# Denominators as products of two factors, one of them in PSUM, and quotients formed in the bank of 1/Q

## The chip, the cores and the metric

The kernel runs on one core of a Trainium2 chip. Its time is device microseconds of one execution; three executions of the kernel before gave 477.53, 478.20 and 479.14 us, so the median is 478.2 us. A profiled execution of its own gave the rows below.

## The reference

Three layers run one after the other. A small attention (a pooled one added to one over a band of seven keys) gives x of 1152 tokens by 512. Then two feed-forward layers follow, each from 512 to 2048 and back to 512:

```
# layer 1
h = x @ w_in
P = a[0] + a[1] * h + a[2] * h * h + a[3] * h * h * h
Q = 1.0 + abs(b[0]) * abs(h) + abs(b[1]) * h * h
y = (P / (Q + 1e-06)) @ w_out
# layer 2
sp = where(h > 20, h, log1p(exp(minimum(h, 20))))
y = (h * tanh(sp)) @ w_out
```

With u = exp(h), tanh(log(1 + u)) is u(u + 2) / (u(u + 2) + 2), so both layers need a quotient whose denominator is D plus a constant, with D = |h|(|b0| + |b1||h|) in layer 1 and D = u(u + 2) in layer 2.

## The kernel before

**Tiles.** The feed-forward work is cut into 81 tiles, 40 in layer 1 and 41 in layer 2. A tile is 128 rows of the hidden dimension, or two such groups side by side, over a block of tokens. In layer 1 the blocks have 256, 256, 256, 192 and 192 tokens and every tile has two row groups, so a tile is 128x512 in the first three blocks and 128x384 in the last two. In layer 2 tiles are 128x512, 128x384 and then 128x512 and 128x256. All products are done as three float16 products (head times head, rest times head, head times rest).

**One tile q passes all engines.** TensorE's `hidden(q)` (L602) fills `h_bank[q % 2]`. ScalarE reads it in `first_reads` (L742 square, L745 scaled magnitude, L748 a cubic coefficient step; in layer 2 L750 the exponential). VectorE's `fraction` works in three parts: in layer 1 L915 (denominator), L922 and L929 (polynomial); in layer 2 L918, L925 (denominator) and L934. ScalarE's `estimate` (L759 logarithm, L761 exponential of its negative) puts about 1/Q in `inv_bank[q % 2]`, which is PSUM. VectorE's `quotient` makes one Newton step and the product in three parts: L943, L947, and L953 or L956. ScalarE's `head` (L769) rounds the result to float16, GpSimd's `rest` (L1061) takes what is left over, and TensorE's `output_first` (L623) or `output_second` (L643) multiplies both with the second weights.

**Order.** Each engine takes its instructions in the order written. TensorE's is output(m), hidden(m + 4), output(m + 1), and so on; hidden(q) waits until VectorE has done part 2 of fraction(q - 2) (`h_done`), output(q) waits for `rest(q)` (`g_rest`). In ScalarE's round m stand first_reads(m), head(m - 2), estimate(m). In VectorE's round m stand fraction part 0 of m, quotient part 0 of m - 1, fraction part 1 of m, quotient part 1 of m - 1, fraction part 2 of m, quotient part 2 of m - 1. Between these pieces `schedule.until(tick)` puts in the attention's pieces and the splitting of weights into head and rest (`head_unit` on ScalarE, L728; `rest_unit` on VectorE, L901, or on GpSimd, L1047 and L1049), at ticks from a table that the change leaves as it is. At the end of a block of layer 1, `leave_y` turns the output banks into the next layer's input: L777 on ScalarE, then L965 on VectorE, for which TensorE's first instruction on these banks (L617) waits.

**The attention** fills the first 55 us, and pieces of it run among the tiles until about 220 us: `put_k` (L684), `put_p` and `put_d` (L668) on ScalarE, pooling and normalising on GpSimd (L1013 to L1037).

Of the kernel before, what the change touches and what calls it, by code (L numbers as in the profile page):

```python
# [10 lines left out]
ALU = mybir.AluOpType  # L11
# [15 lines left out]
def attention_moe_moe(nc, q, k, v, w_in1, w_out1, a, b, w_in2, w_out2, out):  # L27
# [163 lines left out]
    with ExitStack() as ctx:  # L191
# [3 lines left out]
        def sem(name):  # L195
            return ctx.enter_context(nc.semaphore(name))
# [74 lines left out]
        b0_s, b1_abs = coef[:, 10:11], coef[:, 11:12]  # L271
# [35 lines left out]
        h_read = sem("h_read")  # L307
# [356 lines left out]
        def _(act):  # L664
# [68 lines left out]
            def first_reads(q):  # L733

                layer, w = tiles[q][0], width(q)
                ps = h_bank[q % 2][:, 0:w]
                act.wait_ge(h_ready, q + 1)
                if q >= 3:
                    act.wait_ge(g_done, q - 2)
                d, t = den[q % 3][:, 0:w], num[q % 4][:, 0:w]  # L740
                if layer == 0:
                    act.activation(d, ps, ACT.Square, scale=1.0 / HS)  # L742
                    if q >= 2:
                        act.wait_ge(den_done, q - 1)
                    act.activation(ab[q % 2][:, 0:w], ps, ACT.Abs, scale=b0_s).then_inc(h_read, 1)  # L745
                    if q >= 4:
                        act.wait_ge(g_rest, q - 3)
                    act.activation(t, ps, ACT.Identity, scale=a_s[3], bias=a_s[2]).then_inc(t1_done, 1)  # L748
                else:
                    act.activation(d, ps, ACT.Exp, scale=1.0 / HS).then_inc(h_read, 1)  # L750

            def estimate(q):

                layer, w = tiles[q][0], width(q)
                r = inv_bank[q % 2][:, 0:w]
                act.wait_ge(den_done, q + 1)
                if q >= 2:
                    act.wait_ge(nr_done, q - 1)
                act.activation(r, den[q % 3][:, 0:w], ACT.Ln, bias=(one_eps, two)[layer]).then_inc(ln_done, 1)  # L759
                act.wait_ge(ln_done, q + 1)  # L760
                act.activation(r, r, ACT.Exp, scale=-1.0, bias=(0.0, ln_k)[layer]).then_inc(inv_done, 1)  # L761
# [30 lines left out]
            act.activation(b1_abs, b_raw[:, 1:2], ACT.Abs).then_inc(coefs, 1)  # L792
            schedule.until(LAYERS)
            act.wait_ge(coefs, 8)
# [18 lines left out]
        def _(dve):  # L813
# [94 lines left out]
            def fraction(part, q):  # L908

                layer, w = tiles[q][0], width(q)  # L910
                h, d, t = h_bank[q % 2][:, 0:w], den[q % 3][:, 0:w], num[q % 4][:, 0:w]
                if part == 0:
                    dve.wait_ge(h_read, q + 1)
                    if layer == 0:
                        dve.scalar_tensor_tensor(out=d, in0=d, scalar=b1_abs, in1=ab[q % 2][:, 0:w],  # L915
                                                 op0=ALU.mult, op1=ALU.add).then_inc(den_done, 1)
                    else:
                        dve.tensor_scalar(d, d, EXP_20, None, ALU.min).then_inc(clamped, 1)  # L918
                elif part == 1:
                    if layer == 0:  # L920
                        dve.wait_ge(t1_done, q + 1)
                        dve.tensor_tensor(t, t, h, ALU.mult).then_inc(t2_done, 1)  # L922
                    else:
                        dve.wait_ge(clamped, q - N1 + 1)
                        dve.scalar_tensor_tensor(out=d, in0=d, scalar=2.0, in1=d, op0=ALU.add,  # L925
                                                 op1=ALU.mult).then_inc(den_done, 1)
# [10 lines left out]
            def quotient(part, q):  # L937
# [48 lines left out]
            dve.tensor_scalar(b0_s, b_raw[:, 0:1], 1.0 / HS, None, ALU.mult).then_inc(coefs, 1)  # L986
# [5 lines left out]
            dve.wait_ge(coefs, 8)  # L992
# [119 lines left out]
```

## Time and profile before

| what | value |
|---|---|
| median of three executions | 478.2 us |
| profiled execution, its own time | 478.56 us |
| its span, first to last instruction | 476.4 us |
| TensorE busy | 461.9 us, 97% |
| VectorE busy | 398.1 us, 84% |
| ScalarE busy | 306.2 us, 64% |
| GpSimd busy | 214.9 us, 45% |

The profiled execution is 2.16 us longer than its span, and 0.36 us over the median. A busy share is a mean over stages: attention up to about 55 us, layer 1 up to about 290 us, layer 2 after it.

### The profile page before, as it was taken

Reading aid. Unit: us, or ns where it says so; the run is one execution under the profiler, and the core shown is the slowest. Engines: PE = TensorE matmul, PEld = TensorE weight load, DVE = VectorE, ACT = ScalarE, POOL = GpSimd, SP = SyncE. Lnnn points to the kernel's source line nnn. Section 1 sums busy time; section 2 is a strip of 40 time slices with the busy share of each in tenths; the row PEclk is TensorE's granted clock in tenths of the full one; section 3 lists DMA queues with packets and bytes.
Section 4 is the critical chain, followed back from the end, with each engine's and each line's share of the span. In section 5 each row is a group of like instructions: output and inputs, shape, how many; then the busy total and the mean of one; then the engine's idle time right before and its main releaser. Section 6 shows DMA issues by size and latency. Waiting matters only on the chain.

```text
span 476.4 us, 11017 instructions
## 1 busy us (share of the span) xinstructions
PE 461.9 (97%) x4318; PEld 338.3 (71%) x4318; DVE 398.1 (84%) x671; ACT 306.2 (64%) x565; POOL 214.9 (45%) x224
## 2 busy tenths in 40 slices
PE   6999799999999999999999999999999999999996
PEld 5667689898889788899998976444444555557662
DVE  7787799999787887878878788998899888878894
ACT  4477578888566585678877776566545555554542
POOL 5789935579352422117422635762625122212122
PEclk8997899999999999999999999999999999999999
DMA  5989733610801100020200221132000200000101
GB/s 120 247 202 296 159 92 90 161 24 2 190 1 37 24 3 3 1 89 1 89 4 1 89 89 45 45 90 88 0 1 0 90 0 2 0 1 1 66 3 44
DMA packets 46436, 29.71 MB, mean 62 GB/s; under 512 B 31792, under 2 KB 39984, under 8 KB 46384
## 3 DMA queue, kind: packets, MB, share of 16 engines
q1 hardware_dynamic: 45168, 28.71, 22.3%
q8 instruction: 34, 0.56, 0.5%
q10 hardware_dynamic: 1216, 0.30, 0.3%
q14 instruction: 18, 0.15, 0.1%
HBM read 26.64 MB, written 2.36 MB: 61 GB/s over the span
## 4 chain that ended last, share of the span: by engine, by line
PE 77%; POOL 11%; DVE 4%; ACT 3%; issue 3%; DMA 1%; SPq 0%; ACTq 0%; POOLq 0%
PE bank L602 33%; PE bank L643 18%; PE bank L623 17%; PE bank L565 3%; POOL g_l L1061 2%; POOL w L1049 2%; PE bank L509 1%; POOL work L1047 1%; DMA late<-in_k 1%; POOL late L1013 1%; POOL late L1037 1%; POOL late L1049 1%; PE bank L552 1%; ACT late L684 1%; POOL raw L1047 1%
## 5 line engine op out<-in xcount | busy, mean ns | idle before, releaser
L1061 POOL TENSOR_TENSOR g_l<-work,g_h 128x512 f16<-128x512 f32 (+2 forms) x81 | 90.4, 1116 | 212.0 <-ACT g_h L769 179.1
L602 PE MATMUL bank<-x_h,w 128*128 128x256 f16 (+1 forms) x640 | 102.5, 264 | 2.7 <-DVE work L929 2.7
L623 PE MATMUL bank<-g_h,w 128*128 128x256 f16 (+1 forms) x640 | 101.3, 262 | 0.5 <-POOL g_l L1061 0.4
L602 PE MATMUL bank<-x_h,late 128*128 128x512 f16 (+2 forms) x384 | 96.9, 326 | 0.0
L759 ACT ACTIVATE bank<-work,coef 128x512 f32<-128x512 f32 (+2 forms) x81 | 52.3, 646 | 64.3 <-DVE work L925 63.1
L643 PE MATMUL bank<-late,g_h 128*128 128x512 f16 x288 | 92.1, 379 | 0.1
L602 PE MATMUL bank<-x_l,w 128*128 128x256 f16 (+1 forms) x320 | 84.6, 264 | 0.0
L623 PE MATMUL bank<-g_l,w 128*128 128x256 f16 (+1 forms) x320 | 83.8, 262 | 0.0
L602 PEld LDWEIGHTS bank<-x_h,w 128*128 128x128 f16 x640 | 61.4, 99 | 8.5 <-DVE work L929 2.9
L623 PEld LDWEIGHTS bank<-g_h,w 128*128 128x128 f16 x640 | 60.8, 98 | 8.1 <-issue 2.1
L602 PE MATMUL bank<-x_l,late 128*128 128x512 f16 (+2 forms) x192 | 62.6, 326 | 0.0
L602 PEld LDWEIGHTS bank<-x_h,late 128*128 128x128 f16 x384 | 37.6, 98 | 26.2
L915 DVE SCALAR_TENSOR_TENSOR work<-work,coef 128x512 f32<-128x512 f32 (+1 forms) x40 | 32.1, 803 | 27.1 <-ACT work L745 27.0
L643 PE MATMUL bank<-late,g_l 128*128 128x512 f16 x144 | 54.6, 379 | 0.0
L643 PEld LDWEIGHTS bank<-late,g_h 128*128 128x128 f16 x288 | 28.2, 98 | 33.5 <-POOL g_l L1061 1.4
L943 DVE SCALAR_TENSOR_TENSOR work<-work,bank 128x512 f32<-128x512 f32 (+2 forms) x81 | 50.1, 619 | 0.0
L947 DVE SCALAR_TENSOR_TENSOR work<-work,bank 128x512 f32<-128x512 f32 (+2 forms) x81 | 49.9, 616 | 0.0
L769 ACT ACTIVATE g_h<-work 128x512 f16<-128x512 f32 (+2 forms) x81 | 47.3, 583 | 2.5 <-DVE work L956 2.4
L925 DVE SCALAR_TENSOR_TENSOR work<-work 128x512 f32<-128x512 f32 (+2 forms) x41 | 47.1, 1150 | 0.0
L742 ACT ACTIVATE work<-bank 128x512 f32<-128x512 f32 (+1 forms) x40 | 22.2, 555 | 32.0 <-PE bank L602 26.8
L918 DVE TENSOR_SCALAR work<-work 128x512 f32<-128x512 f32 (+2 forms) x41 | 18.8, 460 | 24.6 <-ACT work L750 24.6
L602 PEld LDWEIGHTS bank<-x_l,w 128*128 128x128 f16 x320 | 31.6, 99 | 2.2
(103 smaller groups left out, 804.9 us busy)
## 6 DMA issues: line engine op xcount, KB each, us to landing
raw<-in_moe_w_in SPq DMA_DIRECT2D x10, 512.0 KB, 5.6
raw<-in_moe_w_out SPq DMA_DIRECT2D x10, 512.0 KB, 4.3
late<-in_k SPq DMA_DIRECT2D x16, 144.0 KB, 4.1
late<-in_v SPq DMA_DIRECT2D x8, 288.0 KB
late<-in_v SPq DMA_DIRECT2D x32, 72.0 KB
out<-w SPq DMA_DIRECT2D x9, 256.0 KB, 2.3
late<-in_moe_w_in SPq DMA_DIRECT2D x4, 512.0 KB, 3.6
late<-in_moe_w_out SPq DMA_DIRECT2D x4, 512.0 KB, 4.5
```

The source lines that it names most:

```text
L602: last = pe.matmul(ps, w_in(l, wp)[:, kk, at], x[:, kk, t0:t0 + n], start=(kk == 0 and wp == 0 and x is x_h), stop=(kk == KD - 1 and wp == 1))
L623: last = pe.matmul(ps, w_out(0, wp)[:, f, 128 * d:128 * (d + 1)], g[q % 4][:, i * n:(i + 1) * n], start=False, stop=(f == FT - 1 and d % 2 ...
L643: last = pe.matmul(y2_bank[row % 4][:, :], g[q % 4][:, i * n + 128 * t:i * n + 128 * (t + 1)], w_out(1, wp)[:, f, :], start=(f == 0 and wp ...
L742: act.activation(d, ps, ACT.Square, scale=1.0 / HS)
L759: act.activation(r, den[q % 3][:, 0:w], ACT.Ln, bias=(one_eps, two)[layer]).then_inc(ln_done, 1)
L769: act.activation(g_h[q % 4][:, 0:w], num[q % 4][:, 0:w], ACT.Copy).then_inc(g_head, 1)
L915: dve.scalar_tensor_tensor(out=d, in0=d, scalar=b1_abs, in1=ab[q % 2][:, 0:w], op0=ALU.mult, op1=ALU.add).then_inc(den_done, 1)
L918: dve.tensor_scalar(d, d, EXP_20, None, ALU.min).then_inc(clamped, 1)
L925: dve.scalar_tensor_tensor(out=d, in0=d, scalar=2.0, in1=d, op0=ALU.add, op1=ALU.mult).then_inc(den_done, 1)
L943: dve.scalar_tensor_tensor(out=d, in0=d, scalar=(Q_ONE, 2.0)[layer], in1=r, op0=ALU.add, op1=ALU.mult).then_inc(nt_done, 1)
L947: dve.scalar_tensor_tensor(out=d, in0=d, scalar=(2.0, 2.0 * K2)[layer], in1=r, op0=ALU.subtract, op1=ALU.mult).then_inc(nr_done, 1)
L1061: pool.tensor_tensor(g_l[q % 4][:, 0:w], num[q % 4][:, 0:w], g_h[q % 4][:, 0:w], ALU.subtract).then_inc(g_rest, 1)
```

## The change

Layer 1's denominator was |b1|(h/HS)² + |b0||h/HS|, from two ScalarE reads of the bank and a VectorE operation on two SBUF tiles. Now ScalarE reads the magnitude |h/HS| once into `ab`, a new ScalarE step `factor` makes |b0| + |b1||h/HS| in the PSUM bank of 1/Q, and VectorE multiplies the two. In layer 2 the exponential goes to `ab`, `factor` adds 2 to it in the same PSUM bank, and VectorE multiplies the clamped value by the clamped sum. The last two parts of the quotient change places: part 1 multiplies the numerator by 1/Q and leaves it in the PSUM bank, part 2 multiplies that by the Newton factor and writes the numerator's tile.

```
-                if q >= 3:
-                    act.wait_ge(g_done, q - 2)
-                d, t = den[q % 3][:, 0:w], num[q % 4][:, 0:w]
+                if q >= 2:
+                    act.wait_ge(den_done, q - 1)
                 if layer == 0:
-                    act.activation(d, ps, ACT.Square, scale=1.0 / HS)
-                    if q >= 2:
-                        act.wait_ge(den_done, q - 1)
-                    act.activation(ab[q % 2][:, 0:w], ps, ACT.Abs, scale=b0_s).then_inc(h_read, 1)
+                    act.activation(size, ps, ACT.Abs, scale=1.0 / HS).then_inc(size_done, 1)
                     if q >= 4:
                         act.wait_ge(g_rest, q - 3)
-                    act.activation(t, ps, ACT.Identity, scale=a_s[3], bias=a_s[2]).then_inc(t1_done, 1)
+                    act.activation(num[q % 4][:, 0:w], ps, ACT.Identity, scale=a_s[3], bias=a_s[2]).then_inc(t1_done, 1)
                 else:
-                    act.activation(d, ps, ACT.Exp, scale=1.0 / HS).then_inc(h_read, 1)
+                    act.activation(size, ps, ACT.Exp, scale=1.0 / HS).then_inc(t1_done, 1)
+
+            def factor(q):
+                layer, w = tiles[q][0], width(q)
+                r, size = inv_bank[q % 2][:, 0:w], ab[q % 2][:, 0:w]
+                if q >= 2:
+                    act.wait_ge(g_done, q - 1)
+                if layer == 0:
+                    act.wait_ge(size_done, q + 1)
+                    act.activation(r, size, ACT.Identity, scale=b1_abs, bias=b0_abs).then_inc(factor_done, 1)
+                else:
+                    act.wait_ge(t1_done, q + 1)
+                    act.activation(r, size, ACT.Identity, bias=two).then_inc(factor_done, 1)
...
                 act.wait_ge(den_done, q + 1)
-                if q >= 2:
-                    act.wait_ge(nr_done, q - 1)
...
                 schedule.until(other_tick(m, ACT_PARTS[1]))
+                if m < NT:
+                    factor(m)
                 if 2 <= m < NT + 2:
                     head(m - 2)
...
                 if part == 0:
-                    dve.wait_ge(h_read, q + 1)
+                    dve.wait_ge(t1_done, q + 1)
                     if layer == 0:
-                        dve.scalar_tensor_tensor(out=d, in0=d, scalar=b1_abs, in1=ab[q % 2][:, 0:w],
-                                                 op0=ALU.mult, op1=ALU.add).then_inc(den_done, 1)
-                    else:
-                        dve.tensor_scalar(d, d, EXP_20, None, ALU.min).then_inc(clamped, 1)
-                elif part == 1:
-                    if layer == 0:
-                        dve.wait_ge(t1_done, q + 1)
                         dve.tensor_tensor(t, t, h, ALU.mult).then_inc(t2_done, 1)
                     else:
+                        dve.tensor_scalar(d, size, EXP_20, None, ALU.min).then_inc(clamped, 1)
+                elif part == 1:
+                    dve.wait_ge(factor_done, q + 1)
+                    if layer == 0:
+                        dve.tensor_tensor(d, size, r, ALU.mult).then_inc(den_done, 1)
+                    else:
                         dve.wait_ge(clamped, q - N1 + 1)
-                        dve.scalar_tensor_tensor(out=d, in0=d, scalar=2.0, in1=d, op0=ALU.add,
+                        dve.scalar_tensor_tensor(out=d, in0=r, scalar=EXP_20 + 2.0, in1=d, op0=ALU.min,
                                                  op1=ALU.mult).then_inc(den_done, 1)
...
                     dve.wait_ge(nt_done, q + 1)
-                    dve.scalar_tensor_tensor(out=d, in0=d, scalar=(2.0, 2.0 * K2)[layer], in1=r, op0=ALU.subtract,
-                                             op1=ALU.mult).then_inc(nr_done, 1)
+                    dve.wait_ge(h_done, q + 1)
+                    if layer == 0:
+                        dve.scalar_tensor_tensor(out=r, in0=t, scalar=a_s[0], in1=r, op0=ALU.add,
+                                                 op1=ALU.mult).then_inc(nr_done, 1)
+                    else:
+                        dve.tensor_tensor(r, t, r, ALU.mult).then_inc(nr_done, 1)
                 else:
                     dve.wait_ge(nr_done, q + 1)
-                    dve.wait_ge(h_done, q + 1)
-                    if layer == 0:
-                        dve.scalar_tensor_tensor(out=t, in0=t, scalar=a_s[0], in1=d,
-                                                 op0=ALU.add, op1=ALU.mult).then_inc(g_done, 1)
-                    else:
-                        dve.tensor_tensor(t, t, d, ALU.mult).then_inc(g_done, 1)
+                    dve.scalar_tensor_tensor(out=t, in0=d, scalar=(2.0, 2.0 * K2)[layer], in1=r, op0=ALU.subtract,
+                                             op1=ALU.mult).then_inc(g_done, 1)
```

TensorE's and GpSimd's instructions and their order stay as they were. Two engines' orders change. The first place is ScalarE around 103 to 108 us of the trace, in layer 1 while the attention still runs. Before (the L684 rows are put_k, `work<-bank` are the first reads, L769 the head of tile m - 2, L759 and L761 the estimate):

```order
L742 ACTIVATE work<-bank 128x512 [waits g_done,h_ready]
L745 ACTIVATE work<-bank,coef 128x512 [waits den_done]
L748 ACTIVATE work<-bank,coef 128x512 [waits g_rest]
L684 ACTIVATE late<-bank 64x288 [waits job_filled]
L684 ACTIVATE late<-bank 64x288
L684 ACTIVATE late<-bank 64x288 [waits job_filled]
L684 ACTIVATE late<-bank 64x288
L769 ACTIVATE g_h<-work 128x512 [waits y_added,g_done]
L759 ACTIVATE bank<-work,coef 128x512 [waits nr_done,den_done]
L761 ACTIVATE bank<-bank 128x512 [waits ln_done]
```

The same place of the changed kernel, whose L757 is the new factor, L777 the head, and L767 and L769 the estimate:

```order
L742 ACTIVATE work<-bank 128x512 [waits den_done,h_ready]
L745 ACTIVATE work<-bank,coef 128x512 [waits g_rest]
L685 ACTIVATE late<-bank 64x288 [waits job_filled]
L685 ACTIVATE late<-bank 64x288
L685 ACTIVATE late<-bank 64x288 [waits job_filled]
L685 ACTIVATE late<-bank 64x288
L757 ACTIVATE bank<-work,coef 128x512 [waits size_done,g_done]
L777 ACTIVATE g_h<-work 128x512 [waits y_added,g_done]
L767 ACTIVATE bank<-work,coef 128x512 [waits den_done]
L769 ACTIVATE bank<-bank 128x512 [waits ln_done]
```

One first read is gone from ahead of put_k, and the factor stands behind it, ahead of the head. The second place is VectorE in the 128x384 tiles of layer 1, one round. Before:

```order
L915 SCALAR_TENSOR_TENSOR work<-work,coef 128x384 [waits h_read]
L943 SCALAR_TENSOR_TENSOR work<-work,bank 128x384 [waits inv_done]
L922 TENSOR_TENSOR work<-work,bank 128x384 [waits t1_done]
L947 SCALAR_TENSOR_TENSOR work<-work,bank 128x384 [waits nt_done]
L929 SCALAR_TENSOR_TENSOR work<-work,coef,bank 128x384 [waits t2_done]
L953 SCALAR_TENSOR_TENSOR work<-work,coef 128x384 [waits h_done,nr_done]
```

The same round of the changed kernel, where L926 is the first step of the polynomial, L932 the denominator, L953 the Newton factor, L959 the numerator times 1/Q, L939 the polynomial's next step and L965 the result:

```order
L926 TENSOR_TENSOR work<-work,bank 128x384 [waits t1_done]
L953 SCALAR_TENSOR_TENSOR work<-work,bank 128x384 [waits inv_done]
L932 TENSOR_TENSOR work<-work,bank 128x384 [waits factor_done]
L959 SCALAR_TENSOR_TENSOR bank<-work,coef,bank 128x384 [waits h_done,nt_done]
L939 SCALAR_TENSOR_TENSOR work<-work,coef,bank 128x384 [waits t2_done]
L965 SCALAR_TENSOR_TENSOR work<-work,bank 128x384 [waits nr_done]
```

The denominator has gone from the first place of the round to the third, behind a wait for the factor, and each of the six now has one operand in PSUM.

## Rows read from the trace of the kernel before

**Rows 1.** Busy time by stretch; the columns are named in the first line.

```profile
core 0: us, PE busy (x) PEld busy (x) DVE busy (x) ACT busy (x) POOL busy (x), PEclk, DMA share, GB/s
...
56.61:472.60 415.99, 413.80 (x3703) 301.13 (x3703) 354.09 (x586) 271.55 (x500) 168.80 (x164) 1.00 0.15 43
```

**Rows 2.** Waits: us in total, times, longest; 56 to 80, 100 to 120, 220 to 280 us.

```profile
PE bank L602 <- DVE work L929: 2.7, 1, 2.7
...
PE bank L623 <- POOL g_l L1061: 0.4, 2, 0.2
...
PE bank L617 <- DVE x_l L965: 1.0, 2, 0.8
```

**Rows 3.** Timeline of ScalarE, a 128x384 tile: start us, us, instruction, idle before.

```profile
269.05 0.49 ACT L742 ACTIVATE work<-bank 128x384 f32<-128x384 f32 x1 [1.04 <-PE bank L602]
269.44 0.57 ACT L745 ACTIVATE work<-bank,coef 128x384 f32<-128x384 f32 x1
269.90 0.67 ACT L748 ACTIVATE work<-bank,coef 128x384 f32<-128x384 f32 x1
...
270.87 0.59 ACT L759 ACTIVATE bank<-work,coef 128x384 f32<-128x384 f32 x1
271.50 0.47 ACT L761 ACTIVATE bank<-bank 128x384 f32<-128x384 f32 x1
273.01 0.49 ACT L742 ACTIVATE work<-bank 128x384 f32<-128x384 f32 x1 [1.04 <-PE bank L602]
```

**Rows 4.** Timeline of VectorE in the same tile.

```profile
270.05 0.62 DVE L915 SCALAR_TENSOR_TENSOR work<-work,coef 128x384 f32<-128x384 f32 x1 [0.88 <-ACT work L745]
270.58 0.55 DVE L943 SCALAR_TENSOR_TENSOR work<-work,bank 128x384 f32<-128x384 f32 x1
271.05 0.55 DVE L922 TENSOR_TENSOR work<-work,bank 128x384 f32<-128x384 f32 x1
```

**Rows 5.** Timeline of ScalarE and VectorE, the first tile of layer 1.

```profile
53.00 0.60 ACT L742 ACTIVATE work<-bank 128x512 f32<-128x512 f32 x1 [3.52 <-POOL w L1049]
...
55.10 0.67 DVE L922 TENSOR_TENSOR work<-work,bank 128x512 f32<-128x512 f32 x1
55.81 0.75 DVE L929 SCALAR_TENSOR_TENSOR work<-work,coef,bank 128x512 f32<-128x512 f32 x1
```

**Rows 6.** Busy time by stretch, TensorE's first tiles behind the wait; columns as in rows 1.

```profile
58.00:60.00 2.00, 2.00 (x13) 1.45 (x12) 2.00 (x3) 1.14 (x3) 1.92 (x3) 0.58 0.76 223
```

**Rows 7.** Timeline of ScalarE, layer 1 with attention.

```profile
105.15 1.67 ACT L684 ACTIVATE late<-bank 64x288 f32<-64x288 f32 x4 [0.66 <-PE bank L487]
106.84 0.63 ACT L769 ACTIVATE g_h<-work 128x512 f16<-128x512 f32 x1
107.38 0.67 ACT L759 ACTIVATE bank<-work,coef 128x512 f32<-128x512 f32 x1
```

**Rows 8.** Timeline of GpSimd in the same stretch.

```profile
107.55 1.16 POOL L1061 TENSOR_TENSOR g_l<-work,g_h 128x512 f16<-128x512 f32 x1 [2.55 <-ACT g_h L769]
...
110.56 2.23 POOL L1013 TENSOR_TENSOR late<-late 72x256 f32<-72x256 f32 x1
...
114.35 1.16 POOL L1061 TENSOR_TENSOR g_l<-work,g_h 128x512 f16<-128x512 f32 x1
115.47 1.18 POOL L1013 TENSOR_TENSOR late<-late 72x256 f32<-72x256 f32 x1
```

**Rows 9.** Timeline of ScalarE and VectorE at the end of two blocks.

```profile
224.83 1.08 ACT L777 ACTIVATE x_h<-bank 128x512 f16<-128x512 f32 x2
225.97 1.28 DVE L965 SCALAR_TENSOR_TENSOR x_l<-bank,x_h 128x512 f16<-128x512 f32 x2
258.39 0.87 ACT L777 ACTIVATE x_h<-bank 128x384 f16<-128x384 f32 x2
259.54 1.01 DVE L965 SCALAR_TENSOR_TENSOR x_l<-bank,x_h 128x384 f16<-128x384 f32 x2
```

**Rows 10.** Waits of ScalarE, layer 2, 380 to 455 us.

```profile
ACT bank L759 <- DVE work L925: 27.7, 18, 1.8
```

More of the change, by code:

```diff
@@ L270, in attention_moe_moe @@
         a_s = [coef[:, 6 + i:7 + i] for i in range(4)]
-        b0_s, b1_abs = coef[:, 10:11], coef[:, 11:12]
+        b0_abs, b1_abs = coef[:, 10:11], coef[:, 11:12]
         one_eps, two, ln_k = coef[:, 12:13], coef[:, 13:14], coef[:, 14:15]
@@ L306, in attention_moe_moe @@
         h_ready = sem("h_ready")
-        h_read = sem("h_read")
+        size_done = sem("size_done")
+        factor_done = sem("factor_done")
         h_done = sem("h_done")
@@ L735, in first_reads @@
                 layer, w = tiles[q][0], width(q)
[L736 removed]
+                ps, size = h_bank[q % 2][:, 0:w], ab[q % 2][:, 0:w]
                 act.wait_ge(h_ready, q + 1)
[L738 to L740 removed]
+                if q >= 2:
+                    act.wait_ge(den_done, q - 1)
                 if layer == 0:
[L742 to L745 removed]
+                    act.activation(size, ps, ACT.Abs, scale=1.0 / HS).then_inc(size_done, 1)
                     if q >= 4:
                         act.wait_ge(g_rest, q - 3)
[L748 removed]
+                    act.activation(num[q % 4][:, 0:w], ps, ACT.Identity, scale=a_s[3], bias=a_s[2]).then_inc(t1_done, 1)
                 else:
[L750 removed]
+                    act.activation(size, ps, ACT.Exp, scale=1.0 / HS).then_inc(t1_done, 1)
[10 more added lines that the diff above has]
+                    act.activation(r, size, ACT.Identity, bias=two).then_inc(factor_done, 1)
             def estimate(q):
@@ L791, in _ @@
             act.wait_ge(coef_loaded, 32)
-            act.activation(b1_abs, b_raw[:, 1:2], ACT.Abs).then_inc(coefs, 1)
+            act.activation(coef[:, 10:12], b_raw, ACT.Abs).then_inc(coefs, 1)
             schedule.until(LAYERS)
-            act.wait_ge(coefs, 8)
+            act.wait_ge(coefs, 7)
             for u in EARLY:
@@ L911, in fraction @@
                 h, d, t = h_bank[q % 2][:, 0:w], den[q % 3][:, 0:w], num[q % 4][:, 0:w]
+                r, size = inv_bank[q % 2][:, 0:w], ab[q % 2][:, 0:w]
                 if part == 0:
-                    dve.wait_ge(h_read, q + 1)
+                    dve.wait_ge(t1_done, q + 1)
                     if layer == 0:
-                        dve.scalar_tensor_tensor(out=d, in0=d, scalar=b1_abs, in1=ab[q % 2][:, 0:w],
-                                                 op0=ALU.mult, op1=ALU.add).then_inc(den_done, 1)
-                    else:
-                        dve.tensor_scalar(d, d, EXP_20, None, ALU.min).then_inc(clamped, 1)
-                elif part == 1:
-                    if layer == 0:
-                        dve.wait_ge(t1_done, q + 1)
                         dve.tensor_tensor(t, t, h, ALU.mult).then_inc(t2_done, 1)
                     else:
+                        dve.tensor_scalar(d, size, EXP_20, None, ALU.min).then_inc(clamped, 1)
[4 more added lines that the diff above has]
+                    else:
                         dve.wait_ge(clamped, q - N1 + 1)
-                        dve.scalar_tensor_tensor(out=d, in0=d, scalar=2.0, in1=d, op0=ALU.add,
+                        dve.scalar_tensor_tensor(out=d, in0=r, scalar=EXP_20 + 2.0, in1=d, op0=ALU.min,
                                                  op1=ALU.mult).then_inc(den_done, 1)
@@ L991, in _ @@
             schedule.until(LAYERS)
-            dve.wait_ge(coefs, 8)
+            dve.wait_ge(coefs, 7)
             for m in range(NT + LAG):
```

1 line of the change is left out of this document (removed).

## The prediction

> **What bounds the kernel now.** I read four views in this order: the busy time by stretch, who TensorE waits for, the timelines of one tile on ScalarE and VectorE, and the places where TensorE does stand still. The first says nearly all: from its first tile behind the attention to its last product TensorE is busy 413.80 of 415.99 us at a granted clock of 1.00 [rows 1], so it idles 2.19 us there, and a faster VectorE can give back no more than this, plus what lies ahead of 56.61. The waits name most of it: 2.7 us ahead of that first stretch (the third tile waits for the first tile's L929), 0.4 us for GpSimd's L1061, 1.0 us for L965 at two block ends [rows 2]. In layer 2 it is ScalarE that waits, 27.7 us in 18 times or 1.5 us each, for VectorE's denominator L925 [rows 10]; TensorE has no wait of note there, so what the change saves at L925 shortens a wait that costs nothing.
>
> The tile's timeline shows the margin. In the 128x384 tiles of layer 1 one tile starts 3.96 us after the other (269.05 to 273.01), and ScalarE then stands 1.04 us until TensorE has the next bank ready [rows 3]. TensorE sets the pace there.
>
> **The change part by part.**
>
> *ScalarE, the round of a tile.* Before, the logarithm's denominator came from the first VectorE operation of the round, and ScalarE did L748 and the head meanwhile, so its round was only its own work: from 269.05 to the start of L761 at 271.50 and some 0.39 more, 2.84 us [rows 3]. Now the logarithm waits for the third VectorE operation. Its path in a 128x384 tile: the magnitude read, 0.39 from start to start; the coefficient step, 0.67 [rows 3]; the handoff from ScalarE to VectorE, 0.04 (L745 ends at 270.01, L915 starts at 270.05) [rows 3, 4]; two VectorE operations with a PSUM operand at 0.47 from start to start (270.58 to 271.05) and the third at 0.55 in full [rows 4]; a handoff back, 0.04; logarithm 0.63 from start to start and exponential, 0.39 to 0.47 [rows 3]. That is 0.39 + 0.67 + 0.04 + 0.47 + 0.47 + 0.55 + 0.04 + 0.63 + 0.39 = 3.65 us, at most 3.73. It stays under 3.96, so the 1.04 us of idle time shrink to about 0.3 and TensorE does not notice. The cover that hid the old denominator is nearly used up, though: every piece put between VectorE's first and third place now delays ScalarE as well.
>
> The factor itself costs ScalarE 0.59 (L759, the only row from SBUF into PSUM, with one pointer) to 0.67 (L748, with two) [rows 3]. It replaces one first read of 0.57 in layer 1 and is new in layer 2. It starts about 0.95 us into the round and is done by 1.6, while VectorE reaches the product at 0.39 + 0.67 + 0.04 + 0.94 = 2.04: it is hidden. It stands ahead of the head. In layer 1 a read has gone from ahead of it, so the head comes 0.1 later; in layer 2 some 0.6 later, and what waits behind the head is GpSimd and only then TensorE, which waits for it nowhere in layer 2. I cost it at nothing there.
>
> *VectorE.* Two operations of 0.62 with two SBUF inputs become 0.55 ones with a PSUM input [rows 4], and layer 2's L925 goes from over a microsecond to about 0.68. A PSUM output of VectorE has no row; the nearest are 0.55 and 0.62 of the same shape [rows 4], so it is between 0.1 below and 0.1 above what stands there; I take 0.55. VectorE's round gets shorter, not TensorE's. Cost nothing, gain nothing. On the size of a PSUM operand, "VectorE: DVE Perf Modes" of the Trainium skill (the section on the TRN2 errata) has a fixed part of 120 cycles for a PSUM source against 58 for SBUF. By that rule each moved operation would be an estimated 0.065 us dearer and the round would be 3.8 to 3.9 us, nearly at the pace. The trace disagrees: 0.55 with PSUM against 0.62 without [rows 4].
>
> *The start.* Before, from L742's start at 53.00 to L929's end at 56.56 it took 3.56 us, then TensorE started at 56.61 [rows 1, 5]. Now: first read 0.49 and coefficient step 0.78 (0.39 and 0.67 of the 128x384 tile [rows 3], each made longer by 0.11, the difference of L742 at the two widths, 0.60 and 0.49 [rows 3, 5]), 0.04 handoff, L926 and the product at 0.67 each and L939 at 0.75 [rows 5], less twice the 0.08 by which neighbours overlap: 3.24, so 0.3 us earlier. But TensorE's clock is then at half: 0.58 from 58 to 60 us [rows 6], the 1.2 GHz level for most of it, after it had done nothing for 2.7 us [rows 2]. Work begun earlier in that stretch counts half. I take -0.15 us.
>
> *The crowded stretch.* Around 105 us put_k holds ScalarE from 105.15 to 106.82, and the head follows at 106.84 [rows 7]. The factor now stands between: the head comes about 0.55 later (a 128x512 operation from start to start), GpSimd's L1061 at 108.1 instead of 107.55 [rows 8]. TensorE had waited 0.2 us for it already, so all 0.55 count. The logarithm moves from 107.38 [rows 7] to about 108.25: factor to 107.5, product 0.67, handoff. That is 0.87 us on ScalarE, which it wins back where it waits for TensorE. Next, GpSimd's L1013 took 2.23 us at 110.56 and 1.18 at 115.47 [rows 8], the first beside VectorE operations with two SBUF inputs; without these it is about 1.05 shorter, L1061 at 114.35 comes some 0.5 sooner, and the 0.2 us that TensorE waited for it go. Net 0.55 - 0.22 = +0.33.
>
> *The block ends.* L777 follows the exponential, which comes 3.65 - 2.84 = 0.8 later in the round. At 224.83 that puts the first of its two halves (0.54 each) at 225.65 and VectorE's L965 at 226.3 instead of 225.97: +0.3. At 258.39 it puts L965 at 259.75 instead of 259.54: +0.2 [rows 9]. TensorE waits at both places already [rows 2]. Sum +0.5.
>
> *Sum.* -0.15 + 0.33 + 0.5 = +0.7 us on the profiled execution's 478.56, 479.2. That execution was 0.36 above the median shown, so I forecast 478.9 us, no change. What the measurement can tell from no change is about 0.3%, here 476.8 to 479.6.
>
> **The rivals.**
>
> *Slower: the delay is paid in every crowded round (20%).* Put_k, put_d or the splitting of a weight stand between the first reads and the factor, or between VectorE's first and third place, in many rounds up to 290 us. If TensorE pays the 0.55 us not in one round but in six, this is 5 x 0.55 = 2.8 us more: 481.7. For it: the margin of a round falls from 1.04 to 0.3 [rows 3], so a delay is won back slowly. Against: TensorE's products run three tiles behind, and it now waits at few places [rows 2]. It decides once a delay of ScalarE lasts longer than about a microsecond, twice in a row.
>
> *Slower: the round itself exceeds the pace (8%).* It takes 0.3 us more than I summed, from pointers, waits for a write into PSUM, or slower products. Each 0.1 over 3.96 costs the 16 tiles of 128x384 1.6 us; at 4.2, 3.8 us: 482.7.
>
> *Faster: GpSimd and VectorE stop holding each other up (12%).* L1013 at 2.23 against 1.18 [rows 8] shows the size. If TensorE then loses the waits for L1061 and L965, 1.4 us [rows 2], beside the 0.3 of the start, and my two additions do not come, the time is 476.5. "SBUF — State Buffer" of the Trainium skill (the section on who interferes with whom) states the rule: a VectorE instruction with two SBUF inputs contends with a GpSimd one that reads SBUF, with at most one (outside the modes with two ports) it does not. The trace agrees as far as the 2.23 and 1.18 us go. Against its worth: TensorE has hardly anything left to lose.
>
> *Faster: the clock does not fall (5%).* TensorE's idle time ahead of 56.61 gets 0.3 us shorter, and should its clock stay at 2.4 GHz, the 0.42 that row 58 to 60 lacks [rows 6] comes back; taken over 56.6 to 60 that is 1.4 us: 477.5. Against: 2.4 of the 2.7 us remain.
>
> *That the change doesn't do what it says:* VectorE's share does fall, by about 0.07 us times two per tile of layer 1 and 0.5 in layer 2, and no time comes from it. This is the forecast (55%).
>
> **How the numbers follow.** The forecast's own range is 477.8 to 479.8; with the rivals on both sides the range is 476.6 to 481.8. Faster by more than the bound: most of the port rival, a little of the clock's and of the forecast's edge, 0.16. Slower: 0.28 of the two rivals and some of the forecast's upper edge, 0.31. Same: 0.53.
>
> **What would show it.** VectorE's busy time falls by 20 us or more, ScalarE's rises by 20 or more (41 factors in layer 2 at 0.6). ScalarE's idle time ahead of L742 in the 128x384 tiles falls from 1.04 to about 0.3, and the start to start stays 3.96; a longer one proves the round rival. TensorE starts its third tile at 56.3. L1061 near 108.1 and L965 near 226.3 and 259.75 carry the additions. If TensorE's idle time between its third tile and its last product is over 4 us, the forecast is wrong on the slow side; if it is under 1 us, on the fast side.

## The result and the profile after

Twenty executions of the changed kernel had a median of 481.08 us (479.27 to 483.25), twenty of the kernel before beside them 479.23 us (477.50 to 481.08; the three shown ahead of the prediction, median 478.2, were on the quick side). The ratio is 1.0039 with a 95% interval of 1.0024 to 1.0053: slower by 0.39%, or 1.9 us. I had forecast no change, 478.9 us, with 31% for slower. The measured 481.08 us lies in the whole range (476.6 to 481.8), but above the 479.6 us up to which I would have called it no change and above the forecast's own range (477.8 to 479.8): it is the side that I thought less likely. About 1 us of the distance is the kernel before, whose twenty executions were that much slower than the three that I had reckoned with; the rest is the change.

The profiled execution took 481.16 us with a span of 479.2. TensorE's stretch from its third tile to its last product answers to [rows 1] (columns as there), the second row being that of a second profile of the same kernel:

```profile
57.20:475.35 418.15, 414.15 (x3703) 301.69 (x3703) 318.60 (x586) 305.73 (x543) 157.80 (x164) 1.00 0.15 42
```

```profile
57.11:475.25 418.14, 414.16 (x3703) 301.64 (x3703) 318.36 (x586) 305.61 (x543) 157.56 (x164) 1.00 0.15 42
```

TensorE does the same 3703 products and idles 4.00 us among them (3.98 in the second profile) instead of 2.19. VectorE's busy time there fell by 35 us, from 354.09 to 318.60 (some 21 of them where layer 2's L925 stood), ScalarE's rose by 34, and neither moved the end by itself. Besides the 1.81 us of idle time the stretch holds 0.35 us more of busy time (414.15 against 413.80) for the same products; behind the longer wait at the start TensorE's clock was low for longer (last section). The other views say where the 1.8 us are. TensorE's waits from 50 us on (us in total, times, longest):

```profile
PE bank L603 <- DVE work L939: 5.0, 1, 5.0
PE bank L618 <- DVE x_l L975: 1.4, 2, 0.9
PE bank L624 <- POOL g_l L1070: 0.9, 1, 0.9
PE bank L553 <- ACT late L669: 0.4, 1, 0.4
PE bank L520 <- DVE late L848: 0.4, 1, 0.4
PE bank L644 <- POOL g_l L1070: 0.2, 1, 0.2
PE bank L477 <- DVE late L839: 0.2, 1, 0.2
```

Against [rows 2]: the block ends wait 1.4 us instead of 1.0, GpSimd's g_l 0.9 once instead of 0.2 twice, and three waits are new, L520 and L477 (attention products whose banks VectorE's pieces must empty) and L644 (the last tiles). The 0.4 us of L553 were there before too. That is +0.4, +0.5 and +0.8, 1.7 of the 1.8 us.

The first row, the third tile's wait, is the start, and it has to be read with care. The tile's first read on ScalarE, which stands ahead of everything that the change touches but the reads themselves, began at 53.83 instead of 53.00 us [rows 5]:

```profile
53.83 0.60 ACT L742 ACTIVATE work<-bank 128x512 f32<-128x512 f32 x1 [3.80 <-POOL w L1058]
```

From that read to the third tile, at 57.20, it is 3.37 us now and was 3.61 before (53.00 to 56.61), 0.24 less. The 3.37 came back within 0.01 us in all six other profiles of kernels that keep the changed order on VectorE, so this gain is real. But in the experiments the first read starts anywhere from 51.9 to 56.5 us, so the attention ahead of it differs by more from one execution to another than the whole effect. The spans of two profiles (476.4 and 479.2) must not be compared; TensorE's stretch can be.

The round of a 128x384 tile, which answers to [rows 3] and [rows 4]. ScalarE (L757 is the factor, L767 the logarithm):

```profile
254.32 0.49 ACT L742 ACTIVATE work<-bank 128x384 f32<-128x384 f32 x1 [0.27 <-PE bank L603]
...
258.28 0.49 ACT L742 ACTIVATE work<-bank 128x384 f32<-128x384 f32 x1 [0.26 <-PE bank L603]
258.67 0.67 ACT L745 ACTIVATE work<-bank,coef 128x384 f32<-128x384 f32 x1
259.23 0.68 ACT L757 ACTIVATE bank<-work,coef 128x384 f32<-128x384 f32 x1
...
260.88 0.58 ACT L767 ACTIVATE bank<-work,coef 128x384 f32<-128x384 f32 x1 [0.54 <-DVE work L932]
261.50 0.47 ACT L769 ACTIVATE bank<-bank 128x384 f32<-128x384 f32 x1
```

VectorE, with the first operation that writes PSUM, L959:

```profile
259.37 0.55 DVE L926 TENSOR_TENSOR work<-work,bank 128x384 f32<-128x384 f32 x1 [0.96 <-ACT work L745]
259.84 0.55 DVE L953 SCALAR_TENSOR_TENSOR work<-work,bank 128x384 f32<-128x384 f32 x1
260.30 0.55 DVE L932 TENSOR_TENSOR work<-work,bank 128x384 f32<-128x384 f32 x1
260.77 0.62 DVE L959 SCALAR_TENSOR_TENSOR bank<-work,coef,bank 128x384 f32<-128x384 f32 x1
```

ScalarE's idle time ahead of a tile is 0.26 us, where it was 1.04, and the logarithm now waits 0.54 us for the product. One tile still starts 3.96 us after the other (254.32 to 258.28). The round is as forecast, and it does not set the pace. What was wrong is the crowded stretch, where pieces of other work stand inside the rounds.

### The profile page after: what moved, and what is told of

Its sections match the earlier page's. It is cut to its first block, busy times and chain, and to the rows that moved or that the text cites. A ratio compares the mean times of both kernels' runs of the same rounds, so it can differ in the third digit from the quotient of the medians.

```text
span 479.2 us, 11099 instructions
## 1 busy us (share of the span) xinstructions
PE 459.6 (96%) x4318; PEld 336.9 (70%) x4318; DVE 363.2 (76%) x670; ACT 339.8 (71%) x606; POOL 203.2 (42%) x224
## 4 chain that ended last, share of the span: by engine, by line
PE 70%; POOL 10%; issue 8%; ACT 6%; DVE 3%; DMA 1%; SPq 0%; POOLq 0%; ACTq 0%
PE bank L603 30%; PE bank L644 16%; PE bank L624 15%; POOL g_l L1070 3%; PE bank L566 2%; POOL w L1058 2%; ACT late L685 1%; POOL work L1056 1%; PE bank L510 1%; DMA late<-in_k 1%; ACT work L742 1%; POOL late L1025 1%; PE bank L470 1%; PE bank L531 1%; ACT work L745 1%
## 5 line engine op out<-in xcount | busy, mean ns | idle before, releaser
L644 PE MATMUL bank<-late,g_h 128*128 128x512 f16 x288 | 92.0, 379 | 0.2 <-POOL g_l L1070 0.2
L767 ACT ACTIVATE bank<-work,coef 128x512 f32<-128x512 f32 (+2 forms) x81 | 52.1, 643 | 45.1 <-DVE work L932 29.9
L644 PE MATMUL bank<-late,g_l 128*128 128x512 f16 x144 | 54.6, 379 | 0.0
L926 DVE TENSOR_TENSOR work<-work,bank 128x512 f32<-128x512 f32 (+1 forms) x40 | 25.3, 631 | 38.0 <-ACT work L745 38.0
L644 PEld LDWEIGHTS bank<-late,g_h 128*128 128x128 f16 x288 | 28.2, 98 | 32.8 <-POOL g_l L1070 0.7
L953 DVE SCALAR_TENSOR_TENSOR work<-work,bank 128x512 f32<-128x512 f32 (+2 forms) x81 | 50.3, 621 | 0.0
L965 DVE SCALAR_TENSOR_TENSOR work<-work,bank 128x512 f32<-128x512 f32 (+2 forms) x81 | 50.2, 620 | 0.0
L777 ACT ACTIVATE g_h<-work 128x512 f16<-128x512 f32 (+2 forms) x81 | 46.5, 574 | 1.0 <-DVE work L965 1.0
L747 ACT ACTIVATE work<-bank 128x512 f32<-128x512 f32 (+2 forms) x41 | 22.3, 545 | 32.6 <-PE bank L603 32.4
L624 PEld LDWEIGHTS bank<-g_l,w 128*128 128x128 f16 x320 | 31.3, 98 | 2.3
```

Source lines behind the costliest of these rows:

```text
L624: last = pe.matmul(ps, w_out(0, wp)[:, f, 128 * d:128 * (d + 1)], g[q % 4][:, i * n:(i + 1) * n], start=False, stop=(f == FT - 1 and d % 2 ...
L644: last = pe.matmul(y2_bank[row % 4][:, :], g[q % 4][:, i * n + 128 * t:i * n + 128 * (t + 1)], w_out(1, wp)[:, f, :], start=(f == 0 and wp ...
L747: act.activation(size, ps, ACT.Exp, scale=1.0 / HS).then_inc(t1_done, 1)
L777: act.activation(g_h[q % 4][:, 0:w], num[q % 4][:, 0:w], ACT.Copy).then_inc(g_head, 1)
L953: dve.scalar_tensor_tensor(out=d, in0=d, scalar=(Q_ONE, 2.0)[layer], in1=r, op0=ALU.add, op1=ALU.mult).then_inc(nt_done, 1)
L965: dve.scalar_tensor_tensor(out=t, in0=d, scalar=(2.0, 2.0 * K2)[layer], in1=r, op0=ALU.subtract, op1=ALU.mult).then_inc(g_done, 1)
```

## The experiments

Every kernel was timed in five rounds beside the kernel before. The "theories" are the explanations that each text ahead of a run names. For each I also give TensorE's idle time between its third tile and its last product, from the same view of its own profile, because the start does not enter it.

| kernel | ratio to before (95%) | idle, us |
|---|---|---|
| before | 1 | 2.19 |
| changed kernel, again | 1.0028 (1.0010 to 1.0045) | 3.98 |
| order of the quotient alone | 0.9989 (0.9971 to 1.0007) | 2.37 |
| denominators alone | 1.0032 (1.0013 to 1.0051) | 3.90 |
| factor ahead of the pieces | 1.0026 (1.0003 to 1.0049) | 3.32 |
| product of the factors first | 1.0004 (0.9989 to 1.0019) | 2.85 |
| layer 2 alone | 0.9998 (0.9982 to 1.0015) | 2.46 |
| factor behind the head | 1.0040 (1.0022 to 1.0057) | 4.61 |
| weight pieces behind the product | 1.0014 (0.9994 to 1.0033) | 3.21 |
| before, 20 idle products | 0.9980 (0.9961 to 0.9999) | 2.25 |
| changed, 20 idle products | 1.0030 (1.0011 to 1.0049) | 4.02 |
| before, 28 idle products | 0.9991 (0.9975 to 1.0008) | 2.18 |
| product first, 28 idle products | 0.9989 (0.9971 to 1.0007) | 2.88 |

The idle times come from rows like these, the stretch less the first busy time: order of the quotient alone, denominators alone, factor ahead of the pieces, product first, layer 2 alone, factor behind the head, weight pieces behind the product.

```profile
57.38:473.50 416.12, 413.75 (x3703) 301.33 (x3703) 349.02 (x585) 271.51 (x499) 161.09 (x164) 1.00 0.15 42
```

```profile
56.09:474.00 417.91, 414.01 (x3703) 301.52 (x3703) 322.45 (x585) 305.86 (x542) 162.31 (x164) 1.00 0.15 43
```

```profile
57.02:474.45 417.43, 414.11 (x3703) 301.66 (x3703) 318.43 (x585) 305.62 (x542) 157.44 (x164) 1.00 0.15 42
```

```profile
56.57:474.00 417.43, 414.58 (x3703) 301.93 (x3703) 317.47 (x585) 306.51 (x540) 157.13 (x163) 0.99 0.15 43
```

```profile
60.15:474.70 414.55, 412.09 (x3703) 300.60 (x3703) 329.14 (x585) 298.32 (x540) 163.85 (x164) 1.00 0.15 43
```

```profile
58.62:476.02 417.40, 412.79 (x3703) 300.63 (x3703) 322.63 (x585) 299.26 (x542) 154.04 (x164) 1.00 0.15 43
```

```profile
55.38:472.16 416.78, 413.57 (x3703) 301.55 (x3703) 319.12 (x585) 306.06 (x542) 156.02 (x164) 1.00 0.15 43
```

**The changed kernel again.** No edit.

> The changed kernel once more, for a second profile. Theory A (the longer ScalarE round): TensorE's waits at the crowded places come back: about 0.9 us for the g_l near 111 us, two new waits of 0.2 to 0.4 us for attention pieces on VectorE between 88 and 97 us, 1.4 us at the two block ends; ratio 1.003 to 1.005. Theory B (the start): what was seen is mostly the third tile's wait of 5.0 us and a longer time at 1.2 GHz, which differ from run to run; then this profile shows a start near 56.5 us, a span near 477.5 us and the same small waits.

The waits came back to a tenth (1.4, 0.9, 0.4, 0.2, 0.2 us), so they belong to the kernel. Both profiles had the late start as well, and theory B had forecast an early one. Theory A holds for the waits; theory B is not refuted for the size of the start by this run.

**The order of the quotient alone**, on the kernel before: its first part as it was, then

```
-  d = (d - 2) * r;  t = (t + a0) * d
+  r = (t + a0) * r;  t = (d - 2) * r        # and estimate waits for g_done instead of nr_done
```

> The old denominators with the new order of the quotient, its product left in the bank of 1/Q. Theory A: no difference from before (ratio 0.999 to 1.001), since the logarithm waits for nothing later than before. Theory C (writing into PSUM, or waiting for g_done, is what costs): the whole +0.4%.

0.9989, not distinguishable from before, idle 2.37. One wait of 0.5 us for x_l, where layer 2 begins, is new in its profile and not in the changed kernel's; one of the two for g_l (0.2) is gone. Writing PSUM from VectorE and waiting for `g_done` cost nothing that shows. Theory C is out.

**The denominators alone**: the changed kernel with the old two last parts of the quotient.

```
-                if q >= 2:
-                    act.wait_ge(g_done, q - 1)
+                if q >= 2:
+                    act.wait_ge(nr_done, q - 1)
```

> The new denominators and the factor step with the old order of the quotient. Theory A: all of the loss, ratio 1.003 to 1.005, with the same waits as the changed kernel. Theory C: 1.000.

All of it, within the noise: 1.0032, idle 3.90 us, and the changed kernel's list of waits (1.4, 0.9, 0.4, 0.3, 0.2, 0.2).

**The factor ahead of the pieces.**

```
                 if m < NT:
                     first_reads(m)
+                    factor(m)
                 schedule.until(other_tick(m, ACT_PARTS[1]))
-                if m < NT:
-                    factor(m)
```

> The changed kernel with the factor step right behind the first reads, ahead of the attention's pieces that stood between them on ScalarE. The head then waits no longer behind put_k for the factor, and the denominator is ready earlier in the crowded rounds. Theory A: the wait for g_l near 111 us falls from 0.9 to about 0.3 us and the time by 0.5 to 1 us, to a ratio of 1.001 to 1.003. Theory B: no difference from the changed kernel, 1.004.

The wait for g_l went from 0.9 to 0.2 us, as forecast, and idle time from 3.98 to 3.32; the others stayed. The timed ratio, 1.0026, is too coarse to tell 0.7 us. So 0.7 us hang on the factor's place ahead of the head behind put_k, and 1.1 us on something else.

**The product of the factors first.** ScalarE: magnitude, factor, coefficient step. VectorE in layer 1:

```
 part 0:  wait factor_done;  d = size * r     # was: wait t1_done; t = t * h
 part 1:  wait t1_done;      t = t * h        # was: wait factor_done; d = size * r
```

> The factor step right behind the magnitude read, and on VectorE the product of the two factors in the first place of layer 1's round, as the old denominator was; ahead of the polynomial's first step. Theory A (the loss is the place of the denominator, not its cost): TensorE's idle time between its third tile and its last product goes back from 3.9 to 2.0 to 2.5 us, with the waits at the block ends near 1.0 us; ratio 0.998 to 1.001. Theory D (a further ScalarE step is what costs, wherever it stands): idle time stays over 3.3 us, ratio 1.003.

```profile
PE bank L618 <- DVE x_l L977: 1.4, 2, 1.0
PE bank L624 <- POOL g_l L1072: 0.5, 2, 0.3
```

The two waits for VectorE's pieces are gone and g_l costs 0.5 us; the block ends keep their 1.4. Idle time is 2.85, not the 2.0 to 2.5 expected, and the ratio 1.0004, no longer told from before. The ScalarE step is the same one as in the changed kernel, so theory D, by which idle time stays over 3.3 wherever the step stands, falls: places cost, not the step. Two places changed at once, though. By the run before this one the factor's is worth about 0.7 us and the denominator's so about 0.5. The block ends stay in this kernel, by its timeline, because VectorE's round starts a little later there (its first operation waits for the factor and starts 1.29 us behind the magnitude read, 257.96 against 256.67, where it was 1.00 [rows 3, 4]).

**Layer 2 alone.** Layer 1 as before, layer 2 as in the changed kernel.

> The change in layer 2 alone; layer 1 as before. Theory A: TensorE has no wait of note in layer 2, so nothing but the 0.2 us at the end that the changed kernel's last tiles show; idle time 2.1 to 2.4 us, ratio 0.999 to 1.001. If layer 2 has a part in the loss: idle time over 2.6 us.

0.9998. The one new wait is the 0.2 us of L644 in the last tiles. In 380 to 455 us ScalarE's waits changed as follows, in this kernel and the same in the changed one, against [rows 10]:

```profile
ACT work L752 <- PE bank L603: 17.0, 17, 1.5
ACT bank L768 <- DVE work L938: 4.9, 18, 0.5
```

The 27.7 us of waiting for the denominator turned into waiting for TensorE: the change does what it says in layer 2, and no wait of TensorE depended on it.

**The factor behind the head.**

```
+                if 2 <= m < NT + 2:
+                    head(m - 2)
                 if m < NT:
                     factor(m)
-                if 2 <= m < NT + 2:
-                    head(m - 2)
```

> The changed kernel with the factor step behind the head instead of ahead of it. The head, and so the g_l that TensorE waits for near 111 us, comes 0.5 us sooner, the denominator 0.5 us later. If the head's delay is the path: the wait of 0.9 us falls to about 0.3 us and idle time to 3.3 us, as with the factor early. If the late denominator is the path: the waits for VectorE's pieces and at the block ends (0.4, 0.2, 1.4 us) grow, and idle time is 4 us or more; in the 128x384 tiles the round would reach 3.65 + 0.1 to 0.3 us, hardly idle.

```profile
PE bank L618 <- DVE x_l L975: 1.5, 2, 1.0
PE bank L553 <- ACT late L669: 0.8, 1, 0.8
PE bank L531 <- ACT late L669: 0.8, 1, 0.8
...
PE bank L624 <- POOL g_l L1070: 0.2, 1, 0.2
```

Both expectations came true for their part: the wait for g_l fell to 0.2 us, and others grew or appeared (L531, L553, L477), 4.61 us in all. In this order the later denominator costs more than the sooner head brings. These new waits are for ScalarE's attention pieces (L669, L685) rather than, as expected, for VectorE's.

**The weight pieces behind the product.** Where only pieces that split a weight stood between VectorE's first and third place, they come two places later.

```
+                    if part == 1:
+                        ahead = [e for e in schedule.todo[schedule.done:] if e[0] < tick]
+                        if ahead and all(e[1] is weight_rest for e in ahead):
+                            tick = -math.inf
```

> The changed kernel, where VectorE's pieces that split a weight (L911) and that stood alone between the first and the third place of a round come two places later, behind the product of the factors and L959; in layer 1 that is the one at 79.6 us and two in the 128x384 tiles. The attention's pieces stay where they are. If the piece at 79.6 us is what made the logarithm 1.1 us later at 81.5 us and so the pooling of the keys near 89 us: TensorE's waits for L839 (0.2 us) and L848 (0.4 us) shrink or go, idle time 3.3 to 3.7 us instead of 3.95, the g_l wait (0.9) and the block ends (1.4) stay; ratio 1.002 to 1.0035. If another piece did it: the same waits as the changed kernel, 3.9 us.

In the changed kernel the piece L911 stood behind L953, and L932, the product for which the logarithm waits, behind it. VectorE and ScalarE there:

```profile
79.63 1.22 DVE L911 SCALAR_TENSOR_TENSOR w<-raw,w 128x1024 f16<-128x1024 f32 x1
80.77 0.68 DVE L932 TENSOR_TENSOR work<-work,bank 128x512 f32<-128x512 f32 x1
```

```profile
81.48 0.69 ACT L767 ACTIVATE bank<-work,coef 128x512 f32<-128x512 f32 x1 [1.87 <-DVE work L932]
```

From there ScalarE worked without a pause up to its put_k at 87.34, and VectorE's pooling of the keys, which needs put_k, ended too late for TensorE's L477:

```profile
87.34 1.66 ACT L685 ACTIVATE late<-bank 64x288 f32<-64x288 f32 x4
```

```profile
89.03 0.46 DVE L839 TENSOR_REDUCE late<-bank 128x72 f32<-128x288 f32 x1 [0.32 <-ACT late L685]
```

With the piece moved the logarithm waits 0.73 us instead of 1.87, and put_k, which ran at 80.16 and 84.43, has time left:

```profile
78.37 0.69 ACT L767 ACTIVATE bank<-work,coef 128x512 f32<-128x512 f32 x1 [0.73 <-DVE work L932]
...
84.43 1.67 ACT L685 ACTIVATE late<-bank 64x288 f32<-64x288 f32 x4
```

```profile
PE bank L618 <- DVE x_l L975: 1.4, 2, 0.9
PE bank L624 <- POOL g_l L1075: 0.9, 1, 0.9
...
PE bank L644 <- POOL g_l L1075: 0.2, 1, 0.2
```

L477 and L520 wait no more, idle time is 3.21, 0.8 less and just below the 3.3 to 3.7 forecast; the ratio, 1.0014, is told neither from before nor from the changed kernel. In layer 1 three pieces moved, but the other two stand at 264.7 and 277.9 us of the changed kernel's trace, long after the two waits (89.6 and 97.2 us). So one piece of 1.22 us in the wrong place of one round made both.

Moving the attention's pieces behind the product as well (VectorE's limit for part 1 at 0.56 instead of 0.93) gives no time: in that order the engines end up waiting for one another for ever, one of them for the factor.

**Idle products at the start.** 20 or 28 products of 128x256 into a bank that is free then, ahead of the third tile's wait.

```
+                if q == 2:
+                    for _ in range(20):
+                        pe.matmul(banks[4][:, 0:256], idle[:, 0:128], idle, start=True, stop=True)
```

> The kernel before with 20 idle products of 128x256 on TensorE ahead of its wait for the third tile, where it does nothing for 2.7 to 5.3 us and is then granted half the clock for 3 to 4 us. They write a bank that nobody uses then. Theory E (the start's clock follows TensorE's idling and hides part of every comparison): no low clock behind 56 us, the third tile takes 2.7 us instead of 4.3, and the time falls by 1.2 to 1.9 us, ratio 0.996 to 0.9975, with a narrower spread. If the clock has another cause: 1.000, or slower by what the idle products hold up.

> The changed kernel with the same 20 idle products. Theory E: the clock's part is the same in both kernels and the path's part stays, so against the kernel before it is at 0.999 to 1.001, and 0.35% above the kernel before with the idle products. If the changed kernel's loss were the clock's doing, the two with idle products would be equal.

> The kernel before with 28 idle products ahead of the third tile's wait instead of 20, to cover more of the executions in which the wait is 5 us. Theory E: third tile at the full clock in more executions, ratio 0.996 to 0.9985, at or below that with 20. Where the wait is only 2.7 us they hold the third tile up by some 0.3 us.

> The product of the factors in VectorE's first place, with the 28 idle products. Idle time 2.8 us as without them, third tile at the full clock; ratio 0.997 to 1.000, 0.1% above the kernel before with the same idle products.

In the profile of the kernel before with 20 of them TensorE stood nowhere at the start, and the clock stayed at 1.00, the 2.4 GHz level, against [rows 6]:

```profile
56.00:58.00 2.00, 2.00 (x20) 1.79 (x19) 1.98 (x2) 1.39 (x3) 1.92 (x3) 1.00 0.65 102
58.00:60.00 2.00, 2.00 (x62) 1.78 (x59) 2.00 (x5) 1.72 (x4) 1.92 (x3) 1.00 1.06 391
```

In the changed kernel's the wait was still 2.7 us behind them, and the clock fell as it does without:

```profile
58.00:60.00 2.00, 1.83 (x9) 1.29 (x10) 1.13 (x3) 1.97 (x5) 1.92 (x3) 0.56 0.77 279
```

With 28 of them the picture is as mixed. In the product-first kernel's profile 0.8 us of wait were left and the clock stayed at 1.00; in the kernel before's 2.1 us were left and it fell to 0.50 from 58 to 60 us.

So theory E held for the clock in two profiles of four. The kernel before with 20 is at 0.9980, less of a gain than the 0.9960 to 0.9975 expected and with an interval that ends at 0.9999; with 28, which should have been as good or better, it is at 0.9991. Of a dozen ratios one that just clears 1 proves little: what idle products give on average is open. With 28 the product-first kernel (0.9989) and the kernel before (0.9991) can't be told apart; I had expected 0.1% between them.

The changed kernel with 20 stays at 1.0030, but its clock fell all the same, so this run doesn't say whether the clock has a part in the loss. The order of the quotient alone speaks against a large one: its profile had the wait (5.3 us) and the low clock (0.50, 0.50 and 0.78 from 56 to 62 us) of the changed kernel, and 0.9989 with 2.37 us of idle time. Which clock the timed executions had without a profile isn't on record by stretch.

## Why the prediction was off

The forecast was a sum of small terms, and each can be looked up.

*The start* held: 0.24 us earlier against the 0.3 worked out. I had counted 0.15 of it. The third tile's 57.20 instead of the 56.3 of the forecast is the attention, 0.83 us later in this execution.

*ScalarE's round* held closely. Idle time ahead of a tile 0.26 us (about 0.3 said), the factor 0.68 (0.59 to 0.67), the product 0.55, the write into PSUM 0.62 with its pointer, no more than its kin. From the magnitude read to the start of the exponential it took 3.22 us, where my sum has 3.26. The rival in which the round exceeds the pace did not come. One reading of mine was wrong without harm: I set 0.55 us for a PSUM input against 0.62 for two SBUF inputs, but the 0.62 also has a pointer (a coefficient read from SBUF instead of a constant). For the two-SBUF-input product L956 of the same shape it is 0.54 us, 16 times on average, the same as with one input in PSUM. What made such operations dear is what my rival on GpSimd and VectorE names, that they hold each other up, and it is larger than I saw. L925 took 1.04 us where GpSimd's L1061 had begun just before it:

```profile
400.88 1.04 DVE L925 SCALAR_TENSOR_TENSOR work<-work 128x384 f32<-128x384 f32 x1
```

```profile
400.60 0.91 POOL L1061 TENSOR_TENSOR g_l<-work,g_h 128x384 f16<-128x384 f32 x1 [2.98 <-ACT g_h L769]
```

In the last tiles, at 128x256, it took 1.41 us beside an L1061 (462.31) and 0.41 where it began first (465.71). With one input in PSUM it takes 0.55 at 128x384. So that rival's mechanism was there, worth most of VectorE's 35 us, and still brought nothing, because TensorE did not wait for VectorE there.

*The block ends* held: 1.0 to 1.4 us, +0.4 against +0.5. L785, the L777 of before, starts 3.61 us behind the round's first read at the first of them (224.45 to 228.06) instead of 2.83 (222.00 to 224.83), 0.8 later as worked out. That this later start makes the wait is read from the traces. Product first starts it 3.16 us behind (222.88 to 226.04), but there VectorE's own round is the limit, so no run shows the two apart.

*The wait for g_l* near 110 us held in its mechanism: put_k itself comes 2.08 us later than before (107.23 against 105.15), the head behind it 2.75 (109.59 against 106.84), and the 0.67 between them is the factor's time. I said +0.55 for the first of the two waits and -0.22 for the second, 0.33 in sum. The first went from 0.2 to 0.9, the second vanished: +0.5. ScalarE and GpSimd of the changed kernel, against [rows 7] and [rows 8]:

```profile
107.23 1.67 ACT L685 ACTIVATE late<-bank 64x288 f32<-64x288 f32 x4 [1.23 <-PE bank L488]
108.80 0.77 ACT L757 ACTIVATE bank<-work,coef 128x512 f32<-128x512 f32 x1
109.59 0.63 ACT L777 ACTIVATE g_h<-work 128x512 f16<-128x512 f32 x1
```

```profile
110.30 1.15 POOL L1070 TENSOR_TENSOR g_l<-work,g_h 128x512 f16<-128x512 f32 x1 [3.28 <-ACT g_h L777]
...
113.30 0.73 POOL L1022 TENSOR_TENSOR late<-late 72x256 f32<-72x256 f32 x1
```

The head follows put_k by 0.69 us (108.90 to 109.59) instead of 0.02. GpSimd's L1022, the L1013 of before, took 0.73 us here and 2.23 there, so the contention is gone, as "SBUF — State Buffer" of the Trainium skill (who interferes with whom) has it: VectorE has no two-SBUF-input operation left beside it. The 1.18 us that I took for the undisturbed length was disturbed too: L915 ran beside it (115.98, 1.21 us). What this bought is at most the second wait's 0.2 us.

*The step that failed* is in the part on the crowded stretch: I followed one round to its end and priced the 0.87 us by which the logarithm moves at nothing, because ScalarE "wins back where it waits for TensorE". In the round at 80 us the delay came from VectorE, where a weight piece of 1.22 us stood between the first and third place, and ScalarE found no wait for TensorE to win it back in up to put_k at 87.34; TensorE then stood twice, 0.6 us in all. I had named this ("every piece put between VectorE's first and third place now delays ScalarE as well") and priced it only as a rival, in six rounds at 0.55 us each. It was paid behind one, as the run with the weight piece moved shows, and it cost TensorE those 0.6 us (0.8 by the idle time that came back), where my sum had nothing.

*The tail* was costed at nothing ("TensorE, which waits for it nowhere in layer 2") and took 0.2 us: in the last tiles TensorE waits for g_l once (L644), with layer 2 alone as well. That the factor ahead of the head makes this wait is likely and was not tested.

The sum by measured terms is -0.24 for the start and 4.00 - 2.19 = +1.81, together +1.6 us or 0.33% of 479.2 us; the two timings say 0.39% (0.24 to 0.53) and 0.28% (0.10 to 0.45). By the same terms I had +0.7 us. The four terms that I priced were right in sign; the crowded stretch lacked the late logarithm's 0.6 us, the first wait for g_l was 0.15 too small, the tail's 0.2 us was missing, and with them the sum crossed the bound between no change and slower. My sign of being wrong on the slow side was an idle time over 4 us; it came out at 4.00 and 3.98. That 481.08 us lies inside the range is owed to the rivals' prices that widened it, not to the sum.

## What to carry to other kernels

When a value that the next engine waits for moves from the first place of a round to the third, price everything that a schedule may put between these places, not the two operations alone; look through the crowded stretch round by round. In a kernel whose bound engine is 99% busy, work taken off the others can give back at most that engine's idle time, here 2.19 us, and can lose more: 35 us less on VectorE gave nothing. And compare the bound engine's idle time between two fixed instructions, which agreed to 0.02 us in two profiles of the same kernel, while the spans of the kernel before ran from 474.9 to 478.0 us beside the runs with 28 idle products, more than the whole effect.

## What was not expected

Known before the change, but easily missed: ScalarE's steps cost more with every pointer operand: 0.49 us with none, 0.57 with one, 0.67 with two at 128x384 [rows 3], and the new factor took 0.68 with two. TensorE's clock behind its wait at the start differs between profiles. Before, it was at 0.58 from 58 to 60 us [rows 6] and at 1.00 from 60; in the changed kernel, after a wait of 5.0 us, at 0.50 and still at 0.77 in the next slice:

```profile
58.00:60.00 2.00, 2.00 (x12) 1.41 (x10) 1.16 (x3) 1.88 (x4) 1.92 (x3) 0.50 0.83 251
60.00:62.00 2.00, 2.00 (x22) 1.47 (x20) 2.00 (x4) 1.02 (x2) 2.00 (x2) 0.77 0.36 127
```

With layer 2 alone TensorE stood 2.1 us there and the clock stayed at 1.00; the kernel before with 28 idle products stood 2.1 us too and it fell to 0.50. So the length of that wait by itself doesn't tell.
